# Scores of six chunks by one stacked fp32r matmul a head, in a gated-memory attention kernel

## What is computed

```python
for t in range(S):
    m_new = np.maximum(f_gate[:, :, t] + m, i_gate[:, :, t])
    f_stab, i_stab = np.exp(f_gate[:, :, t] + m - m_new), np.exp(i_gate[:, :, t] - m_new)
    C = f_stab * C + i_stab * (v_t outer k_t)
    n = f_stab * n + i_stab * k_t
    y[:, :, t] = sigmoid(o_gate) * (C @ q_t) / np.maximum(abs(n @ q_t), 1.0)
x = y as (1536 tokens, 320)
x = (sigmoid(x @ w_gate) * (x @ w_val)) @ w_out      # 320 -> 1536 -> 320
x = ((x @ w_a) * (x @ w_b)) @ w_out2                 # 320 -> 1536 -> 320
```

## Time and profile before

| what | value |
|---|---|
| median of 3 runs | 474.76 us (474.63 to 476.84) |
| the profiled execution, whole | 474.71 us |
| its span, first to last instruction | 472.9 us |
| TensorE matmul / weight load busy | 464.6 / 407.5 us |
| DVE, ACT, POOL busy | 176.7, 185.4, 113.3 us |

### The profile page before, as it was taken

The page is one execution under the profiler, slowest core; times in us unless marked ns, Lnnn a source line. Parts: engine busy times, 40 slices in busy tenths (PEclk is TensorE's granted clock), DMA queues, the critical chain, the costliest instruction groups (busy, mean ns, idle before and its releaser), DMA issues.

```text
span 472.9 us, 6554 instructions
## 1 busy us (share of the span) xinstructions
PE 464.6 (98%) x2534; PEld 407.5 (86%) x2534; DVE 176.7 (37%) x339; ACT 185.4 (39%) x348; POOL 113.3 (24%) x104
## 2 busy tenths in 40 slices
PE   8989999999999999999999999999999999999997
PEld 5878888888988888988888888888888888888886
DVE  8866353433443434334222244222232222322223
ACT  5954756362543527224433453222232222322222
POOL 4586675824031120000554442000000000000000
PEclk9999999999999999999999999999999999999999
DMA  5877755322313152000222300000010000100001
GB/s 154 243 246 228 215 155 148 112 75 74 98 51 105 44 192 98 1 0 2 96 94 94 106 36 1 0 1 0 1 56 1 0 1 0 57 1 1 0 1 55
DMA packets 18118, 33.67 MB, mean 71 GB/s; under 512 B 2385, under 2 KB 12340, under 8 KB 18088
## 3 DMA queue, kind: packets, MB, share of 16 engines
q1 hardware_dynamic: 17752, 32.25, 22.0%
q10 hardware_dynamic: 176, 0.66, 0.5%
q0 software_dynamic: 160, 0.35, 0.3%
HBM read 31.17 MB, written 2.04 MB: 70 GB/s over the span
## 4 chain that ended last, share of the span: by engine, by line
PE 94%; POOL 3%; DMA 1%; DVE 1%; issue 0%; SPq 0%; POOLq 0%; DVEq 0%
PE bank L533 54%; PE bank L550 27%; PE bank L434 4%; PE bank L459 4%; PE bank L450 1%; POOL w_lo_end L1042 1%; PE bank L485 1%; PE bank L473 1%; PE bank L515 1%; PE bank L407 1%; DMA arow<-a_lo 1%; POOL w_lo_mid L1042 1%; POOL x_n L1014 1%; POOL w_lo L1042 0%; DMA i_row<-i_in 0%; DMA vk<-vk_in 0%
## 5 line engine op out<-in xcount | busy, mean ns | idle before, releaser
L879 DVE TENSOR_TENSOR h_ff<-bank,s_ff 128x512 f32<-128x512 f32 x72 | 49.8, 692 | 191.0 <-PE bank L533 190.8
L533 PE MATMUL bank<-xt,w_hi 128*128 128x512 f32 x360 | 118.7, 395 | 0.5 <-issue 0.5
L697 ACT CAST h_hi<-h_ff 128x512 fp32r<-128x512 f32 x72 | 44.5, 618 | 135.2 <-DVE h_ff L879 132.2
L690 ACT ACTIVATE s_ff<-bank 128x512 f32<-128x512 f32 x72 | 43.1, 598 | 135.7 <-PE bank L533 135.6
L533 PE MATMUL bank<-xt,w_lo 128*128 128x512 f32 x216 | 84.5, 391 | 0.0
L533 PEld LDWEIGHTS bank<-xt,w_hi 128*128 128x128 f32 x360 | 65.7, 188 | 12.2 <-issue 0.9
L885 DVE TENSOR_TENSOR h_lo<-h_ff,h_hi 128x512 fp32r<-128x512 f32 x72 | 51.7, 718 | 54.2 <-ACT h_hi L697 54.2
L533 PE MATMUL bank<-xt,w_hi_end 128*128 128x512 f32 x180 | 59.3, 394 | 0.0
L533 PE MATMUL bank<-xt,w_hi_mid 128*128 128x512 f32 x180 | 59.3, 394 | 0.0
L533 PEld LDWEIGHTS bank<-xt,w_lo 128*128 128x128 f32 x216 | 40.6, 188 | 8.8
L550 PE MATMUL bank<-w_hi,h_hi 128*128 128x320 f32 x144 | 45.1, 313 | 0.0
(11 more groups left out here) (114 smaller groups left out, 658.2 us busy)
## 6 DMA issues: line engine op xcount, KB each, us to landing
w_raw<-w_in SPq DMA_DIRECT2D x24, 544.0 KB, 3.8
vk<-vk_in SPq DMA_DIRECT2D x12, 344.0 KB, 3.4
levels<-a_scratch SPq DMA_DIRECT2D x7, 512.0 KB
k<-kq_in SPq DMA_DIRECT2D x11, 180.0 KB
y<-rows_t SPq DMA_DIRECT2D x12, 160.0 KB, 1.9
q<-kq_in SPq DMA_DIRECT2D x10, 180.0 KB
q_blk<-kq_in SPq DMA_DIRECT2D x22, 60.0 KB
osig_b<-o_in SPq DMA_DIRECT2D x8, 160.0 KB, 3.2
```

What stands on the lines that cost most here:

```text
L533: mm = pe.matmul(up_bank(u, gv)[:, :], w_part(low, f, (gv * 3 + kt) * P, P), xt[:, xb * TOK + g * TG:xb * TOK + (g + 1) * TG], start=(j == ...
L690: act.activation(s_ff[u % 2][:, :], up_bank(u, 0)[:, :], ACT.Sigmoid if u < UNITS // 2 else ACT.Copy).then_inc(act_s, 1)
L697: act.copy(h_hi[u % 2][:, :], h_ff[u % 2][:, :]).then_inc(act_h, 1)
L879: dve.tensor_tensor(h_ff[u % 2][:, :], up_bank(u, 1)[:, :], s_ff[u % 2][:, :], ALU.mult).then_inc(dve_h, 1)
```

## The change

Chunks 6 to 11 (STACKED = 6) get their scores in another way. For each head one fp32r matmul of 128 columns has 120 rows as three thirds of 40: the keys' thirds are high, low, high, the queries' thirds high, high, low, so that the sum over the rows is the sum of the three products. SP loads keys and queries of a chunk each three times under each other (`load_both`, six transfers in place of four, 960 KB in place of 340). For keys and then for queries, ACT makes a signed rounded copy, minus in the third that is to be low (`part_high`, into the space of `q_blk`), and DVE adds the raw value there (`stack_low`), in place. The masks `low_rows` and `sign` are made once, ahead of the loop. To make room, the weights of ACT go into `pt` itself (no `wt`), `s_ff` is one buffer (gate waits for the product before), and half of `consts` is no longer loaded.

```diff
-        consts = sb("consts", [P, 2 * P])
-        ident = consts[:, 0:P]
+        ident = sb("ident", [P, P])
...
+        both = [landing.enter_context(nc.sbuf_tensor(f"{x}_both", [TRI, HEADS * P], F32)) for x in "kq"]
+        landing.close()
+        stack = [sb(f"{x}_stack", [TRI, HEADS * P], F32R) for x in "kq"]
+        sign, low_rows = sb("sign", [TRI, 2]), sb("low_rows", [TRI, 2])
+        part = q_blk[0][:, :].bitcast(F32R)
...
-        wt = sb("wt", [P, HEADS * P])
...
-        s_ff = [sb(f"s_ff{i}", [P, TG]) for i in range(2)]
+        s_ff = [sb("s_ff", [P, TG])] * 2
...
+            def load_both(n):
+
+                wait(sp, pe_s, 2 * n if n > STACKED else 0)
+                for x in range(2):
+                    for j, k in ((0, 3), (1, 3), (2, 2)):
+                        here = slice(3 * j * P, (3 * j + k) * P)
+                        src = kq3_in[n, j * HD:(j + 1) * HD, 3 * x * P:(3 * x + k) * P].unsqueeze(0)
+                        sp.dma_start(both[x][:, here], src.to_broadcast([3, HD, k * P])).then_inc(ld_both[x], 16)
...
-                    load_q(n + 1)
+                    if n + 1 < STACKED:
+                        load_q(n + 1)
+                    else:
+                        load_both(n + 1)
...
             def scores(n, half):
...
-                if n == ALONE - 1:
+                if n >= STACKED:
+                    wait(pe, dve_stack, 2 * (n - STACKED) + 2)
+                elif n == ALONE - 1:
...
+                if n >= STACKED:
+                    for h in range(HEADS // 2):
+                        g = half * HEADS // 2 + h
+                        own = slice((3 * (g % 3) + g // 3) * P, (3 * (g % 3) + g // 3 + 1) * P)
+                        mm = pe.matmul(st[:, h * P:(h + 1) * P], stack[0][:, own], stack[1][:, own],
+                                       start=True, stop=True)
+                    mm.then_inc(pe_s, 1)
+                    return
...
             def weigh(n, half):
-                wait(act, dve_p, 2 * n - 1 + half)
+                wait(act, pe_fv, before(n) + 1)
...
+            def part_high(n, x):
+
+                k = 2 * (n - STACKED) + x
+                act.wait_ge(ld_both[x], 48 * (n - STACKED) + 48)
+                act.wait_ge(dve_sign, 1)
+                act.wait_ge(pe_s, 2 * n)
+                wait(act, dve_stack, k)
+                act.activation(part, both[x][:, :], ACT.Copy, scale=sign[:, x:x + 1]).then_inc(act_part, 1)
...
             def gate(u):
-                wait(act, dve_h, u - 1)
+                wait(act, dve_h, u)
...
             for u in range(UNITS):
+                if k == 0 and n >= STACKED:
+                    part_high(n, 1)
                 gate(u)
...
+                if k == 2 and STACKED <= n + 1 < NCH:
+                    part_high(n + 1, 0)
                 if k == 2:
                     x_high(n)
...
+            def stack_low(n, x):
+
+                dve.wait_ge(act_part, 2 * (n - STACKED) + x + 1)
+                dve.scalar_tensor_tensor(out=stack[x][:, :], in0=both[x][:, :], scalar=low_rows[:, x:x + 1],
+                                         in1=part.bitcast(F32), op0=ALU.mult, op1=ALU.add).then_inc(dve_stack, 1)
...
+            dve.wait_ge(pool_low, 5)
+            dve.tensor_scalar(sign[:, :], low_rows[:, :], -2.0, 1.0, ALU.mult, ALU.add).then_inc(dve_sign, 1)
             for u in range(UNITS):
                 h_low(u)
...
+                if k == 0 and n >= STACKED:
+                    stack_low(n, 1)
+                if k == 2 and STACKED <= n + 1 < NCH:
+                    stack_low(n + 1, 0)
                 if k == 2:
                     x_low(n)
```

More of the change, by code:

```diff
@@ L46 @@
 RING = 3
+STACKED = 6
 LOW = -1.0e30
@@ L139, in build @@
         w_raw = [sb(f"w_raw{i}", [P, WC]) for i in range(RING)]
-        consts = sb("consts", [P, 2 * P])
-        ident = consts[:, 0:P]
+        ident = sb("ident", [P, P])
         osig_b = [sb(f"osig_b{i}", [P, DM]) for i in range(2)]
+        landing = ExitStack()
+        both = [landing.enter_context(nc.sbuf_tensor(f"{x}_both", [TRI, HEADS * P], F32)) for x in "kq"]
[3 more added lines that the diff above has]
+        part = q_blk[0][:, :].bitcast(F32R)
         d_row, m_prev = sb("d_row", [ROWS, CHUNKS]), sb("m_prev", [ROWS, CHUNKS])
-        wt = sb("wt", [P, HEADS * P])
         v_w = [sb(f"v_w{i}", [P, VALL]) for i in range(2)]
@@ L179, in build @@
         ld_q_own = sem("ld_q_own")
+        ld_both = [sem(f"ld_both_{x}") for x in "kq"]
+        act_part, dve_stack, pool_low, dve_sign = (sem(n) for n in ("act_part", "dve_stack", "pool_low", "dve_sign"))
         act_whi, pool_wlo = sem("act_whi"), sem("pool_wlo")
@@ L323, in _ @@
             sp.dma_start(i_row[:, :], i_in).then_inc(ld_gate, 16)
-            sp.dma_start(consts[:, :], consts_in).then_inc(ld_ident, 16)
+            sp.dma_start(ident[:, :], consts_in[:, 0:P]).then_inc(ld_ident, 16)
             sp.wait_ge(dve_zero, 1)
@@ L639, in weigh @@
                     col = n * HEADS + half * HEADS // 2 + h
-                    a = act.activation(wt[:, at:at + P], level, ACT.Exp, scale=-1.0,
+                    a = act.activation(pt[set_of(n)][:, at:at + P], level, ACT.Exp, scale=-1.0,
                                        bias=g_col[:, col:col + 1])
@@ L821, in product @@
                 own = slice(half * HALF, (half + 1) * HALF)
-                dve.tensor_tensor(pt[s][:, own], score_bank(n, half)[:, :], wt[:, own], ALU.mult).then_inc(dve_p, 1)
+                dve.tensor_tensor(pt[s][:, own], score_bank(n, half)[:, :], pt[s][:, own], ALU.mult).then_inc(dve_p, 1)
                 if half and n <= ALONE:
@@ L1098, in _ @@
             w_low(1)
+            pool.memset(low_rows[:, :], 1.0).then_inc(pool_low, 1)
+            pool.wait_ge(pool_low, 1)
+            for x in range(2):
+                pool.affine_select(low_rows[:, x:x + 1], low_rows[:, x:x + 1], [[0, 1]], ALU.is_gt, 0.0,
+                                   base=1 - (x + 1) * HD, channel_multiplier=1).then_inc(pool_low, 1)
+            pool.wait_ge(pool_low, 3)
+            for x in range(2):
+                pool.affine_select(low_rows[:, x:x + 1], low_rows[:, x:x + 1], [[0, 1]], ALU.is_gt, 0.0,
+                                   base=(x + 2) * HD, channel_multiplier=-1).then_inc(pool_low, 1)
             W_AT = {0: (2,), 1: (3, 4), 3: (5, 6), 4: (7, 8), 6: (9, 10), 7: (11,)}
```

## The result

The changed kernel takes **502.92 us** (median of 4 runs, 501.25 to 504.52), the kernel before 474.69 in the runs beside it: ratio **1.0576**, 95% interval 1.0544 to 1.0608. That is 28 us slower, and far outside the forecast of 475.0 (472.0 to 479.0). The profiled execution took 504.52 us, with a span of 502.8 where the earlier trace rows had 472.9; its mean granted clock was 0.969 (0.969 to 0.973 in the four runs).

The account below looks back on a forecast made before the run. The prediction took TensorE (PE), busy in 98% of the span, as the bound. Score matmuls -4.9, waits for the stacks +4.5 and starts after them +0.7 gave +0.3 on 474.71: 475.0 us, range 472.0 to 479.0.

Parts of the forecast that it names:

- the rest, priced at nothing: Mask setup ahead of the loop, weights in pt, one s_ff, and larger loads: all taken to add no time.
- Loads late: Rival: copies in each stacked chunk wait 1 us for DMA, giving 481.0 us; chance 0.04.
- land some 3 us later, into slack of a unit: The q3, i_rep and vk transfers queued behind the new loads: delayed some 3 us, at no cost.
- The score group: PE's eight fp32r score matmuls per chunk, 6 to 11: 0.92 us instead of 1.74, saving 4.9 us if PE never waited.
- the start after a wait: On PE at each stacked chunk's scores: restart plus signal cost 0.11 us a chunk, 0.7 in all.
- The copy: ScalarE's part_high of 120x1024, for keys and for queries: 1.04 us each.
- The sum: VectorE's stack_low of 120x1024, for keys and for queries: 1.22 us each, bounds 1.04 and 1.68.
- The side edits at nothing: Masks made ahead of the loop, weights written into pt, a single s_ff: priced at no time.
- TensorE's waits for the stack: Ahead of the scores in chunks 6 to 11: 1.27, 0.33, 0.97 and three of 0.63, 4.5 us in all.
- the signals: After each PE wait for a stack: 0.05 us for the signal, counted within 0.11 a chunk.
- Longer split chain: Rival: stack_low, on the path twice a chunk, takes up to 1.68 us, giving 480.5 us; chance 0.20.
- No wait at all: Rival: PE never waits for the stacks in chunks 6 to 11, giving 469.8 us; chance 0.06.

Follow-up runs that it names:

- e1_wide: Changed kernel with keys and queries laid out three times by the host, so the transfers' slowest dimension is 120 rows: 478.5 us, ratio 1.0066.
- e2_loads_only: Changed kernel with no chunk stacked, old loads kept, and its slow transfers for chunks 6 to 11 issued in addition, read by nothing: 488.63 us, ratio 1.0259.
- e5_filler: Changed kernel with eleven matmuls that nobody reads ahead of the scores of chunks 6 to 11: 501.51 us, ratio 1.055.
- e4_sum_first: e1_wide with VectorE's queries' sum moved ahead of the hidden product of the same unit: 470.82 us, ratio 0.9895.
- e0_room_only: Changed kernel with no chunk stacked (STACKED = 12), only the edits at the side kept: 475.27 us, ratio 0.9999.
- e6_forty: Changed kernel with each of a chunk's six transfers replaced by three of 40 rows, same inputs: 480.07 us, ratio 1.0095.
- e3_six: e1_wide with the host's rows in six padded groups of 20, so the transfers' slowest dimension is 6: 480.64 us, ratio 1.0112.

## Why the prediction was wrong

- **The step that failed** is in "the rest, priced at nothing": the loads. The prediction counted bytes (1.5 MB in 12 us, 125 GB/s) against the best slices of the earlier trace rows, and put "Loads late" at 0.04 and 1 us a chunk. But the 243 to 246 GB/s there are a rate at which 0.8 and 0.7 of the 16 engines were busy. `load_both`'s own shape, three copies slowest, gave 68 to 75 GB/s at a fifth of the engines, under the 125 that were needed. e1_wide against the changed kernel prices it at 24.4 us. The prediction named the right path ("each us by which they came late would go through gate to PE"); the rate, and with it size and chance of the rival, were wrong.
- **What stands behind on SyncE's queue** was said to "land some 3 us later, into slack of a unit". The prediction named q3, i_rep and vk there and left the weight tiles out, and these had no such slack: they held ScalarE 9.3 us in the changed kernel. e2_loads_only shows 13.4 us with no reader at all.
- **A fall of the clock** was not in the prediction. It came behind the waits. How much time it took by itself stays open (e5_filler).
- **The score group**: 0.92 predicted. By the prediction's own measure (first score matmul to the third up-projection matmul, less two at 0.23) it is 0.90 in e4_sum_first, without a wait, and 1.00 in e1_wide, behind one; the 0.94 to 0.95 read above are to the first up-projection matmul. The difference of 0.10 is the start after a wait, which the prediction had priced apart. **The copy**: 1.04, measured 1.15. **The sum**: 1.22, measured 1.28. **The side edits at nothing**: right (e0_room_only).
- **TensorE's waits for the stack**: 4.5 us predicted; 12.5 in the changed kernel, but 5.9 in e1_wide, where the loads are out of the way. The mechanism is there as described: in chunks 8 to 11 ScalarE's copy of the queries waits for VectorE's sum of the keys (0.7 to 1.1 us), and gate stands behind it. But 5.9 is too little. The profile counts a wait from the modelled end of the matmul before, 0.39 after its start, where the next could have started 0.23 after it. By starts, the scores come 1.7, 0.5, 1.4 and three times 1.1 us late in chunks 6 to 11, 6.8 in all, against 4.5 and 0.3 for the signals. The sizes give most of the difference: 0.11 for each copy and 0.06 for each sum, 0.34 where all four lie on the path, as in chunks 8 to 11.
- **The forecast without its error** would have been e1_wide: 475.0 predicted, 478.5 measured, in the range but on its upper side. Its profiled run took 477.63, 2.9 over that of the kernel before; -5.0 for the matmuls (6 x 0.84), +6.8 for the waits and +0.6 for the starts give +2.4, and 0.5 stays open. e4_sum_first checks it: it removes waits and starts, 7.4 us by this account, and is 7.7 us faster than e1_wide.
- **Longer split chain** (0.20, 480.5): the right kind, and worth some 2 us (7.4 for waits and starts where 5.2 were predicted), not 5.5. What it rested on, a sum held up beside GpSimd, occurs in e1_wide in one sum of twelve (1.75 for 1.28, chunk 6). **No wait at all** (0.06, 469.8): not this kernel, but e4_sum_first is that case and takes 470.8. The prediction followed the chain row by row, and took VectorE's order as given.

## What to carry to other kernels

Price a new transfer by its own access pattern, not by the page's best slice: look up or measure how many DMA engines its slowest dimension lets it use, and compare that rate with the time from issue to need. Then name everything that the same queue issues behind it, weight tiles above all. And where a new operation makes the costliest engine wait, look at what stands ahead of it on its own engine: here, once the transfers were wide, one moved line, with no other work changed, turned a loss of 3 us into a gain of 4.

## What the runs showed that I had not expected

- While one kind of transfer keeps the queue full, the DMA engines' busy share follows how many engines it uses: 0.19 to 0.22 with a slowest dimension of 3, 0.37 to 0.39 with 6, 0.63 to 0.86 with 120 rows. Where the issues set the pace (e6_forty, 0.45 to 0.51) it does not, and the packet counts tell more.
- A slow transfer is slow for its issuer as well: a q_both issue took 0.70 to 2.94 us with 3 copies, 0.41 with 120 rows.
- TensorE's clock fell to half behind waits of 1.8 to 3.8 us, but not behind each of them. Matmuls that filled the waits for the stacks kept it up there and left the time where it was.
- A sum on VectorE that meets a weight split on GpSimd took 2.42 us in place of 1.28 (e4_sum_first).
- Transfers at about 120 GB/s in place of 227 to 262 cost 2 us in all (e3_six against e1_wide); at 68 to 75 GB/s they cost 24. Three points do not give a curve, but the steep part lies where the loads take longer than the time that is there for them.
